# Down-weights in a ring of four and a down-projection two units behind, in a fused gated scan and two MLPs

## Chip, cores and metric

One core of a Trainium2 chip. The metric is the device time of one execution in microseconds (us), as a median of several runs.

## What is computed

```python
# x, f_logit: (1, 6080, 256); lower_bound: (256,)
f = lower_bound + (1 - lower_bound) * sigmoid(f_logit)
for t in range(6080):
    h = f[:, t] * h + (1 - f[:, t]) * x[:, t];  y[:, t] = h
h = y @ w_in1                       # 256 -> 2048
y = maximum(0.01 * h, h) @ w_out1   # leaky, 2048 -> 256
h = y @ w_in2
out = where(h > 0, h, exp(minimum(h, 0)) - 1) @ w_out2   # ELU
```

All of it is float32. The kernel splits each matmul operand in a high and a low part (`_hi`, `_lo`, type fp32r) and makes three matmuls of each product: hi x hi, hi x lo and lo x hi.

## The kernel before

Features lie on the 128 partitions and tokens along the free dimension. The 6080 tokens are cut into 6 pairs of tiles (`PAIRS`); a tile of the first pair has 480 tokens (`N0`), every other one 512 (`BANK`). The 2048 hidden features are 8 pairs of 128-row blocks (`H`, index p). A "step" s multiplies one pair of tiles by one pair of blocks: seven products (Strassen's scheme, `product`) up and eight blocks down (`down11` to `down21`). Steps run over pairs 1 to 5 of the leaky MLP and then over all 6 pairs of the ELU MLP.

The first pair of the first MLP has no steps. Its work is done in 16 **units**, each one tile t and one block pair p, with plain products: `unit_up(i)` is 12 matmuls of 480 columns (2 hidden blocks x 2 feature halves x 3), `unit_down(i)` 12 more into `y_ps`. `unit(i)` gives the order: tile 0 of a block pair comes first and tile 1 two units later, (0,0), (0,1), (1,0), (0,2), (1,1) and so on. TensorE runs `unit_up(i)` and then `unit_down(i-1)`; the last down stands inside step 0, in two halves.

What a unit needs: ACT copies the two PSUM banks to `e` (`unit_pre`), DVE takes the leaky function (`unit_leaky`), ACT writes `g_hi` (`unit_split`), DVE `g_lo` (`g0_ready`). `e`, `g_hi` and `g_lo` have two places, i % 2. ACT's `unit_split(i)` waits for `down0_done >= i - 1`, `unit_up(i)` for the copies of unit i-2.

The weights are split on the way. The raw up-weights of block pair p come to one of three places of `c` (`load_a`), ACT and DVE split them (`split_a`, `a_ready`). The raw down-weights come to the single buffer `w_out_raw` (`load_w_out`), ACT writes `w_out_hi` and DVE `w_out_lo` (`split_w_out`, `w_out_ready`). For the seven products of the steps another load of w_in (`load_w_in`, buffer `w_in_raw`) gets four sums on POOL (`w_sums`) and is split too (`split_w_in`, `w_in_ready`).

All engines are in order. All big loads are issued by SP, in an order written out by hand: `load_w_out(i)` waits for `w_out_ready >= i`, `load_w_in(i)` for `w_in_ready >= i`, `load_a(p)` for `a_ready >= p - 2`; in the loop over i, `load_a(i+1)`, `load_w_out(i)`, `load_w_in(i-2)` follow one another. The scan inputs of pair 1 (`load_scan(1)`) stand ahead of that loop, those of pair 2 (`load_scan(2)`) behind `load_w_in(7)`. On ACT and DVE the small tasks are hung between the unit's own operations in `unit_extra` and `unit_after`, and in a step in `extra`. There, in step 0, ACT has `split_w_in(6)`, `tanh(2,0)`, `tanh(2,1)`, and behind them `split_w(0)` and `copy_sums`, which moves `y_ps` of the first pair to `result`; `down11(0)`, in step 1, waits for that (`y_copied`). The last product of step 0 waits for DVE's `add22`, which stands behind `split11`, and this for the last `unit_down`.

Of the kernel before, what the change touches and what calls it, by code (L numbers as in the profile page):

```python
# [8 lines left out]
def bass_gated_scan__leaky_mlp__elu_mlp(  # L9
# [18 lines left out]
    ALU = mybir.AluOpType  # L28
# [12 lines left out]
    RING = 3  # L41
# [47 lines left out]
    w_in_h, w_out_h = (w_in1, w_in2), (w_out1, w_out2)  # L89

    ctx = ExitStack()
    with ctx:
# [96 lines left out]
        w_out_loaded = sem("w_out_loaded")  # L189
        w_sum_ready = sem("w_sum_ready")  # L190
# [30 lines left out]
        def _(sp):  # L221
# [107 lines left out]
        def _(sc):  # L329
# [22 lines left out]
            def first_gate(n):  # L352
                k, t = FIRST[n]
                f = first_tile(f_in, k, t)
                sc.wait_ge(f0_loaded[n], DMA)
                nc.scalar.activation(f, f, ACT.Tanh, scale=0.5).then_inc(tanh0_ready, 1)
                if n == 0:
                    sc.wait_ge(bound_steps, 2)
                sc.wait_ge(tanh0_ready, n + 1)
                nc.scalar.activation(f, f, ACT.Identity, bias=f_shift[:, k:k + 1], scale=f_scale[:, k:k + 1]  # L360
                                     ).then_inc(forget0_ready, 1)
# [6 lines left out]
            def forget1(k):  # L368
                sc.wait_ge(tanh_ready, k + 1)
# [17 lines left out]
            def split_w_out(i):  # L387
                p = i % H
                sc.wait_ge(w_out_loaded, DMA * (i + 1))
                if i >= H:  # L390
                    sc.wait_ge(out_done, 4 * (LEAKY_STEPS - H + p + 1))
                nc.scalar.copy(w_out_hi[:, p, :], w_out_raw[:, :, :].rearrange("p b c -> p (b c)")
                               ).then_inc(w_out_hi_ready, 1)
# [222 lines left out]
        def _(ve):  # L616
# [503 lines left out]
```

## Time and profile before

| | us |
|---|---|
| median of 3 runs | 1071.63 (1070.43 to 1072.32) |
| the profiled execution | 1072.25 |
| its span | 1070.5 |
| TensorE busy (PE) | 1027.6 (96%) |
| VectorE busy (DVE) | 859.8 (80%) |
| ScalarE busy (ACT) | 620.3 (58%) |

The span runs from the first to the last instruction. PE is TensorE's matmul, PEld its weight load, SP the engine that issues the DMAs. In a row of a timeline the first two numbers are start and duration in us; a bracket at the end tells how long the engine was idle ahead of this operation and who released it. A matmul's duration reaches beyond the start of the next one: the matmuls are pipelined, and the distance of two starts is what one costs.

### The profile page before, as it was taken

What the parts mean: (1) busy time and instruction counts of PE and PEld (TensorE: products, weight loads), DVE (VectorE), ACT (ScalarE), POOL (GpSimd) and SP (SyncE); (2) the same over time, 40 slices, a digit from 0 to 9 for tenths busy, and PEclk for the clock granted to TensorE, in tenths of its full rate; (3) what the DMA queues carried; (4) which work ended last, traced back from release to release, by engine and by line L of the source; (5) the groups of instructions that cost most, each with busy time, mean ns of one, the idle gap of its engine ahead of it and who ended that gap; (6) DMA issues with size and microseconds to landing.
All of it is one profiled execution on the core that took longest, in us unless ns stands there. A gap on an engine that the chain in (4) does not pass through costs nothing.

```text
span 1070.5 us, 12489 instructions
## 1 busy us (share of the span) xinstructions
PE 1027.6 (96%) x4374; PEld 827.3 (77%) x4374; DVE 859.8 (80%) x1118; ACT 620.3 (58%) x953; POOL 43.2 (4%) x69
## 2 busy tenths in 40 slices
PE   8778869999999999999999999999999999999997
PEld 5667648878878887887887888888888888888886
DVE  6356658878888888887999888888888888888775
ACT  5443544554464554455667766767676666666564
POOL 0011200000000000000431000000000000000000
PEclk9899879999999999999999999999999999999999
DMA  4321030030030021010213011011011001001001
GB/s 128 123 59 50 20 126 1 1 118 0 1 118 1 1 79 40 1 57 18 82 59 99 1 40 38 1 40 40 1 40 40 1 27 52 1 1 40 1 1 39
DMA packets 24814, 42.41 MB, mean 40 GB/s; under 512 B 2224, under 2 KB 13488, under 8 KB 24752
## 3 DMA queue, kind: packets, MB, share of 16 engines
q1 hardware_dynamic: 24176, 41.36, 11.4%
q8 instruction: 34, 0.56, 0.2%
q10 hardware_dynamic: 576, 0.26, 0.1%
q14 instruction: 28, 0.23, 0.1%
HBM read 29.16 MB, written 12.45 MB: 39 GB/s over the span
## 4 chain that ended last, share of the span: by engine, by line
PE 84%; DVE 2%; DMA 1%; ACT 1%; issue 0%; SPq 0%; DVEq 0%; ACTq 0%
PE y_ps L967 15%; PE y_ps L969 15%; PE y_ps L968 15%; PE a_ps L958 7%; PE a_ps L960 7%; PE a_ps L959 7%; PE c_ps L960 4%; PE c_ps L958 4%; PE c_ps L959 4%; PE b_ps L960 2%; PE b_ps L958 2%; PE b_ps L959 2%; DMA f_in<-f_logitT 1%; ACT g_hi L487 0%; DVE g_lo L793 0%
## 5 line engine op out<-in xcount | busy, mean ns | idle before, releaser
L967 PE MATMUL y_ps<-g_hi,w_out_hi 128*128 128x512 f32 (+1 forms) x768 | 307.9, 401 | 33.0 <-DVE g_lo L650 19.0
L968 PE MATMUL y_ps<-g_lo,w_out_hi 128*128 128x512 f32 (+1 forms) x768 | 305.7, 398 | 0.0
L969 PE MATMUL y_ps<-g_hi,w_out_lo 128*128 128x512 f32 (+1 forms) x768 | 305.3, 397 | 0.0
L967 PEld LDWEIGHTS y_ps<-g_hi,w_out_hi 128*128 128x128 f32 x768 | 146.8, 191 | 72.9 <-DVE g_lo L650 24.0
L969 PEld LDWEIGHTS y_ps<-g_hi,w_out_lo 128*128 128x128 f32 x768 | 147.0, 191 | 33.7
L968 PEld LDWEIGHTS y_ps<-g_lo,w_out_hi 128*128 128x128 f32 x768 | 147.0, 191 | 32.4
L487 ACT CAST g_hi<-e 128x1024 fp32r<-128x1024 f32 (+1 forms) x88 | 92.1, 1046 | 113.4 <-DVE e L774 111.3
L958 PE MATMUL a_ps<-x_hi,w_in_hi 128*128 128x512 f32 (+1 forms) x352 | 139.3, 396 | 2.7 <-DVE c L736 2.7
L960 PE MATMUL a_ps<-x_hi,w_in_lo 128*128 128x512 f32 (+1 forms) x352 | 139.1, 395 | 0.0
L959 PE MATMUL a_ps<-x_lo,w_in_hi 128*128 128x512 f32 (+1 forms) x352 | 139.1, 395 | 0.0
L793 DVE TENSOR_TENSOR g_lo<-e,g_hi 128x1024 fp32r<-128x1024 f32 (+1 forms) x88 | 107.8, 1225 | 7.0 <-ACT g_hi L487 2.2
L454 ACT ACTIVATE e<-c 128x1024 f32<-128x1024 f32 (+1 forms) x48 | 50.6, 1053 | 75.9 <-DVE c L731 70.1
L438 ACT COPY c<-c_ps 128x512 f32<-128x512 f32 (+1 forms) x88 | 51.4, 584 | 61.5 <-PE c_ps L960 61.5
L726 DVE TENSOR_TENSOR c<-c,b_ps 128x512 f32<-128x512 f32 (+1 forms) x88 | 60.2, 684 | 33.2 <-PE b_ps L960 32.6
L789 DVE TENSOR_TENSOR g_lo<-e,g_hi 128x512 fp32r<-128x512 f32 (+1 forms) x88 | 61.3, 696 | 30.0 <-ACT g_hi L479 30.0
L731 DVE TENSOR_TENSOR c<-c,c_ps 128x512 f32<-128x512 f32 (+1 forms) x88 | 60.3, 685 | 29.1 <-PE c_ps L960 28.9
L958 PEld LDWEIGHTS a_ps<-x_hi,w_in_hi 128*128 128x128 f32 x352 | 66.5, 189 | 18.5 <-DVE c L736 3.1
L960 PEld LDWEIGHTS a_ps<-x_hi,w_in_lo 128*128 128x128 f32 x352 | 66.5, 189 | 15.6
L959 PEld LDWEIGHTS a_ps<-x_lo,w_in_hi 128*128 128x128 f32 x352 | 66.5, 189 | 15.4
L960 PE MATMUL c_ps<-x_hi,w_in_lo 128*128 128x512 f32 (+1 forms) x176 | 69.6, 395 | 0.0
L958 PE MATMUL c_ps<-x_hi,w_in_hi 128*128 128x512 f32 (+1 forms) x176 | 69.6, 395 | 0.0
L959 PE MATMUL c_ps<-x_lo,w_in_hi 128*128 128x512 f32 (+1 forms) x176 | 69.5, 395 | 0.0
(94 smaller groups left out, 1502.0 us busy)
## 6 DMA issues: line engine op xcount, KB each, us to landing
f_in<-f_logitT SPq DMA_DIRECT2D x10, 512.0 KB, 4.9
x_in<-xT SPq DMA_DIRECT2D x10, 512.0 KB, 6.1
mid<-result SPq DMA_DIRECT2D x10, 512.0 KB, 3.5
x_in<-mid SPq DMA_DIRECT2D x5, 1024.0 KB, 5.0
outT<-result SPq DMA_DIRECT2D x10, 512.0 KB, 2.8
w_out_raw<-w_out SPq DMA_DIRECT2D x16, 256.0 KB, 3.1
w_in_raw<-w_in SPq DMA_DIRECT2D x32, 128.0 KB, 2.3
f_in<-f_logitT SPq DMA_DIRECT2D x4, 240.0 KB, 5.0
```

The lines of the kernel that those rows point to most:

```text
L438: nc.scalar.copy(c[:, 2, cols(s)], c_ps[:, cols(s)]).then_inc(snap5_ready, 1)
L487: nc.scalar.copy(g_hi[:, 1:3, cols(s)], e[:, 1:3, cols(s)]).then_inc(hi_w_ready, 1)
L726: nc.vector.tensor_tensor(c[:, 0, cols(s)], c[:, 0, cols(s)], b_ps[:, cols(s)], ALU.add).then_inc(c11_ready, 1)
L731: nc.vector.tensor_tensor(c[:, 1, cols(s)], c[:, 1, cols(s)], c_ps[:, cols(s)], ALU.add).then_inc(c12_ready, 1)
L789: nc.vector.tensor_tensor(g_lo[:, 0, cols(s)], e[:, 0, cols(s)], f32_view(g_hi[:, 0, cols(s)]), ALU.subtract).then_inc(g11_ready, 1)
L793: nc.vector.tensor_tensor(g_lo[:, 1:3, cols(s)], e[:, 1:3, cols(s)], f32_view(g_hi[:, 1:3, cols(s)]), ALU.subtract).then_inc(g_w_ready, 1)
L958: nc.tensor.matmul(out, w_in_hi[:, p, at], hi, start=start, stop=False, skip_group_check=not start)
L959: nc.tensor.matmul(out, w_in_hi[:, p, at], lo, start=False, stop=False, skip_group_check=not start)
L960: return nc.tensor.matmul(out, w_in_lo[:, p, at], hi, start=False, stop=True, skip_group_check=not start)
L967: nc.tensor.matmul(out, w_out_hi[:, p, at], hi, start=(p == 0 and j == 0), stop=False)
L968: nc.tensor.matmul(out, w_out_hi[:, p, at], lo, start=False, stop=False)
L969: last = nc.tensor.matmul(out, w_out_lo[:, p, at], hi, start=False, stop=(p == H - 1 and j == 1))
```

## The change

The raw down-weights of the first MLP get four places in `result` (`OUT_RING`, `raw_out`), which holds nothing until the first sums are copied; these copies now also wait for `w_out_ready >= 8`. SP issues loads 0 to 3 at once and 4 to 7 as places come free, and `load_a` ahead of `load_scan(1)` as far as block pair 6; `load_w_in(7)` goes behind `load_scan(2)`. The order of the units puts tile 0 two units further ahead. `unit_down` comes two units behind `unit_up`, so that the last two stand in step 0. The gate of the first pair (`Identity` with scale and bias) moves from ACT to DVE (`first_forget`), and the small tasks of the first units are ordered anew.

```diff
-    RING = 3
+    RING, OUT_RING = 3, 4
 def unit(i):
-        if i == 0:
-            return 0, 0
-        if i == UNITS - 1:
-            return 1, H - 1
-        return (0, (i + 1) // 2) if i % 2 else (1, i // 2 - 1)
+        if i < 3:
+            return 0, i
+        if i >= UNITS - 3:
+            return 1, i - H
+        return (1, (i - 3) // 2) if i % 2 else (0, i // 2 + 1)
+        def raw_out(i):
+            return result[:, i % OUT_RING // 2, i % 2, :] if i < H else w_out_raw[:, :, :].rearrange("p b c -> p (b c)")
 # SP: load_w_out
-                if i > 0:
+                raw = raw_out(i).rearrange("p (b c) -> p b c", c=D)
+                if i < H:
+                    if i >= OUT_RING:
+                        sp.wait_ge(w_out_ready, i - OUT_RING + 1)
+                    sp.dma_start(raw, w_out1[:, 2 * p:2 * p + 2, :]).then_inc(w_out0_loaded[i % OUT_RING], DMA)
+                else:
                     sp.wait_ge(w_out_ready, i)
-                sp.dma_start(w_out_raw[:, :, :], w_out_h[m][:, 2 * p:2 * p + 2, :]).then_inc(w_out_loaded, DMA)
+                    sp.dma_start(raw, w_out2[:, 2 * p:2 * p + 2, :]).then_inc(w_out_loaded, DMA)
 # SP: order of the loads, behind load_w_out(1)
+            load_w_out(2)
+            load_w_out(3)
+
+            load_a(3)
+            load_a(4)
+            load_w_out(4)
+            load_a(5)
+            load_w_out(5)
+            load_a(6)
             load_scan(1)
+            load_w_out(6)
             load_w_in(0)
-            for i in range(2, H):
-                if i + 1 < H:
-                    load_a(i + 1)
-                load_w_out(i)
-                if i > 2:
-                    load_w_in(i - 2)
-            load_w_in(H - 2)
-            load_w_in(H - 1)
+            load_a(7)
+            load_w_out(7)
+            for i in range(1, H - 1):
+                load_w_in(i)
 # ... and behind load_scan(2), ahead of store(0)
+                if r == 1:
+                    load_w_in(H - 1)
 # ACT: the start
-            first_gate(0)
-            first_gate(1)
+            first_tanh(0)
+            first_tanh(1)
+            first_split(0)
             split_a(0)
-            first_split(0)
-            first_gate(2)
+            first_tanh(2)
+            split_a(1)
             first_split(1)
-            split_a(1)
-            first_gate(3)
+            first_tanh(3)
 # DVE: the gate
+                nc.vector.tensor_scalar(f, f, f_scale[:, k:k + 1], f_shift[:, k:k + 1],
+                                        ALU.mult, ALU.add).then_inc(forget0_ready, 1)
 # ACT: unit_extra (split_a and split_w_out on DVE likewise)
                 if i == 0:
+                    split_a(2)
                     split_w_out(0)
+                if i == 1:
                     first_split(2)
-                elif i == 1:
                     first_split(3)
                     split_w_out(1)
-                    split_a(2)
-                elif i % 2 and (i + 3) // 2 < H:
-                    split_a((i + 3) // 2)
-                elif i % 2 == 0 and i // 2 + 1 < H:
+                    split_a(3)
+                if i == 2:
+                    split_w_out(2)
+                if i >= 3 and i % 2 and (i + 5) // 2 < H:
+                    split_a((i + 5) // 2)
+                if i >= 4 and i % 2 == 0 and i // 2 + 1 < H:
                     split_w_out(i // 2 + 1)
 # DVE: unit_after
                 if i == 0:
                     split_w_out(0)
+                    first_forget(3)
+                    first_input(3)
                     scan(0, 1, 1)
                     first_split(2)
+                    first_split(3)
                 if i == 1:
-                    first_split(3)
+                    split_a(3)
                     save_carry(0)
-                    split_w_out(1)
-                    split_a(2)
+                if i == 2:
+                    split_w_out(2)
 # ACT and DVE, extra(s) and copy_sums(0)
-                if s < 2:
-                    split_w_in(H - 2 + s)
+                if s in (0, 2):
+                    split_w_in(H - 2 + s // 2)
                 if r == 0:
                     sc.wait_ge(down0_done, units_through(t, H - 1))
+                    sc.wait_ge(w_out_ready, H)
 # TensorE: step 0, between A12 and S1; and the loop over the units
                 else:
+                    unit_down(UNITS - 2, (0, 1))
                     pe.wait_ge(pre0, 2 * UNITS)
-                if i > 0:
-                    unit_down(i - 1, (0, 1))
+                if i > 1:
+                    unit_down(i - 2, (0, 1))
```

## Rows read from the trace of the kernel before

**Rows 1.** Stretches: us, then busy us (and count) of each engine, granted clock, DMA

```profile
11.43:125.44 114.01, 92.42 (x372) 76.14 (x373) 66.14 (x73) 52.26 (x82) 12.15 (x24) 0.90 0.20 61
39.42:42.62 3.20, 3.20 (x9) 2.64 (x8) 2.21 (x3) 1.47 (x2) 0.00 (x0) 0.50 0.04 16
125.44:159.19 33.75, 22.05 (x80) 17.01 (x79) 17.42 (x23) 12.78 (x20) 3.98 (x8) 0.80 0.31 107
159.19:1070.40 911.21, 904.38 (x3895) 730.76 (x3893) 771.13 (x1015) 548.36 (x843) 26.33 (x32) 1.00 0.09 32
```

**Rows 2.** Timeline of TensorE without waits; 98.06 to 105.03 is 32 starts

```profile
98.06 0.38 PE L989 MATMUL a_ps<-x_hi,w_in_lo 128*128 128x480 f32 x1
...
105.03 0.38 PE L988 MATMUL c_ps<-x_lo,w_in_hi 128*128 128x480 f32 x1
...
158.49 0.40 PE L958 MATMUL a_ps<-x_hi,w_in_hi 128*128 128x512 f32 x1
...
159.19 0.39 PE L958 MATMUL a_ps<-x_hi,w_in_hi 128*128 128x512 f32 x1
```

**Rows 3.** Timeline of TensorE, units: four of its six restarts after a wait

```profile
19.22 0.67 PE L967 MATMUL y_ps<-g_hi,w_out_hi 128*128 128x480 f32 x1 [2.12 <-DVE w_out_lo L655]
...
38.85 0.77 PE L967 MATMUL y_ps<-g_hi,w_out_hi 128*128 128x480 f32 x1 [6.74 <-DVE g_lo L650]
...
80.64 0.71 PE L967 MATMUL y_ps<-g_hi,w_out_hi 128*128 128x480 f32 x1 [2.09 <-DVE g_lo L650]
...
94.91 0.49 PE L967 MATMUL y_ps<-g_hi,w_out_hi 128*128 128x480 f32 x1 [1.91 <-DVE g_lo L650]
```

**Rows 4.** Timeline of TensorE, steps 0 and 1: its restarts after a wait

```profile
135.11 0.61 PE L958 MATMUL a_ps<-x_hi,w_in_hi 128*128 128x512 f32 x1 [2.69 <-DVE c L736]
...
148.04 0.77 PE L967 MATMUL y_ps<-g_hi,w_out_hi 128*128 128x512 f32 x1 [9.01 <-ACT result L504]
```

**Rows 5.** Waits, 0 to 110 us: engine and operation, releaser, us, times, longest

```profile
ACT w_out_hi L392 <- DMA w_out_raw<-w_out: 27.5, 5, 8.6
```

**Rows 6.** Waits of SP's queue, 0 to 120 us

```profile
SPq L258 <- DVE w_in_lo L621: 70.0, 5, 20.4
```

**Rows 7.** Groups by line, 0 to 160 us: count, busy, mean ns, idle

```profile
L967 PE MATMUL y_ps<-g_hi,w_out_hi 128*128 128x480 f32 x64 | 28.9, 451 | 21.2 <-DVE g_lo L650 19.0 <-DVE w_out_lo L655 2.1
...
L650 DVE TENSOR_TENSOR g_lo<-e,g_hi 128x960 fp32r<-128x960 f32 x16 | 18.9, 1178 | 11.7 <-ACT g_hi L385 11.7
L646 DVE SCALAR_TENSOR_TENSOR e<-e 128x960 f32<-128x960 f32 x16 | 18.5, 1154 | 12.4 <-ACT e L379 12.4
...
L385 ACT CAST g_hi<-e 128x960 fp32r<-128x960 f32 x16 | 15.9, 992 | 10.9 <-DVE e L646 10.9
...
L379 ACT COPY e<-a_ps 128x480 f32<-128x480 f32 x16 | 8.9, 555 | 15.8 <-PE a_ps L989 15.8
...
L655 DVE TENSOR_TENSOR w_out_lo<-w_out_raw,w_out_hi 128x512 fp32r<-128x512 f32 x8 | 5.5, 690 | 24.1 <-ACT w_out_hi L392 24.1
...
L360 ACT ACTIVATE f_in<-f_in,f_shift,f_scale 128x480 f32<-128x480 f32 x4 | 3.2, 788 | 0.2
...
L691 DVE TENSOR_TENSOR_SCAN x_in<-f_in,carry,x_in 128x512 f32<-128x512 f32 x2 | 2.6, 1278 | 0.0
...
L661 DVE TENSOR_SCALAR f_in<-f_in,f_scale,f_shift 128x1024 f32<-128x1024 f32 x2 | 1.6, 810 | 6.1 <-ACT f_in L398 6.1
```

**Rows 8.** Loads of f issued at 25.62, 137.91, 138.84: KB, us to landing

```profile
f_in<-f_logitT SPq DMA_DIRECT2D x1, 512.0 KB, 7.1
...
f_in<-f_logitT SPq DMA_DIRECT2D x1, 512.0 KB, 4.1
...
f_in<-f_logitT SPq DMA_DIRECT2D x1, 512.0 KB, 5.7
```

**Rows 9.** Timeline of ACT in step 0

```profile
142.01 1.06 ACT L398 ACTIVATE f_in<-f_in 128x1024 f32<-128x1024 f32 x1 [7.19 <-DMA f_in<-f_logitT]
...
146.47 1.47 ACT L504 COPY result<-y_ps 128x480 f32<-128x480 f32 x3
```

More of the change, by code:

```diff
@@ L88, in bass_gated_scan__leaky_mlp__elu_mlp @@
     mid_h = mid.rearrange("(k p) s -> p k s", p=P)
-    w_in_h, w_out_h = (w_in1, w_in2), (w_out1, w_out2)
+    w_in_h = (w_in1, w_in2)
     ctx = ExitStack()
@@ L189, in bass_gated_scan__leaky_mlp__elu_mlp @@
         w_out_loaded = sem("w_out_loaded")
+        w_out0_loaded = [sem(f"w_out0_loaded{n}") for n in range(OUT_RING)]
         w_sum_ready = sem("w_sum_ready")
@@ L350, in split_a, with first_tanh @@
                 nc.scalar.copy(w_in_hi[:, p, 0:4 * P], c[:, p % RING, :]).then_inc(a_hi_ready, 1)
-            def first_gate(n):
-                k, t = FIRST[n]
-                f = first_tile(f_in, k, t)
+            def first_tanh(n):
+                f = first_tile(f_in, *FIRST[n])
                 sc.wait_ge(f0_loaded[n], DMA)
                 nc.scalar.activation(f, f, ACT.Tanh, scale=0.5).then_inc(tanh0_ready, 1)
[L357 to L361, printed above, removed]
             def first_split(n):
@@ L368, in forget1 @@
             def forget1(k):
+                if k == 0:
+                    sc.wait_ge(bound_steps, 2)
                 sc.wait_ge(tanh_ready, k + 1)
@@ L388, in split_w_out @@
                 p = i % H
-                sc.wait_ge(w_out_loaded, DMA * (i + 1))
-                if i >= H:
+                if i < H:
+                    sc.wait_ge(w_out0_loaded[i % OUT_RING], DMA * (i // OUT_RING + 1))
+                else:
+                    sc.wait_ge(w_out_loaded, DMA * (i - H + 1))
                     sc.wait_ge(out_done, 4 * (LEAKY_STEPS - H + p + 1))
-                nc.scalar.copy(w_out_hi[:, p, :], w_out_raw[:, :, :].rearrange("p b c -> p (b c)")
-                               ).then_inc(w_out_hi_ready, 1)
+                nc.scalar.copy(w_out_hi[:, p, :], raw_out(i)).then_inc(w_out_hi_ready, 1)
             def tanh(r, k):
@@ L598, in _ @@
                 unit_pre(i, 1)
-                if i != 1:
-                    unit_extra(i)
+                unit_extra(i)
                 unit_split(i)
-                if i == 1:
-                    unit_extra(i)
             for s in range(STEPS):
@@ L627, in split_a, with first_forget @@
                                         ALU.subtract).then_inc(a_ready, 1)
+            def first_forget(n):
+                k, t = FIRST[n]
+                f = first_tile(f_in, k, t)
+                ve.wait_ge(tanh0_ready, n + 1)
+                nc.vector.tensor_scalar(f, f, f_scale[:, k:k + 1], f_shift[:, k:k + 1],
+                                        ALU.mult, ALU.add).then_inc(forget0_ready, 1)
             def first_input(n):
@@ L654, in split_w_out @@
                 ve.wait_ge(w_out_hi_ready, i + 1)
-                nc.vector.tensor_tensor(w_out_lo[:, i % H, :], w_out_raw[:, :, :].rearrange("p b c -> p (b c)"),
+                nc.vector.tensor_tensor(w_out_lo[:, i % H, :], raw_out(i),
                                         f32_view(w_out_hi[:, i % H, :]), ALU.subtract).then_inc(w_out_ready, 1)
@@ L801, in copy_sums @@
                     ve.wait_ge(down0_done, units_through(0, H - 1))
+                    ve.wait_ge(w_out_ready, H)
                 else:
@@ L808, in extra @@
                 r, p = pair_of(s)
-                if s < 2:
-                    split_w_in(H - 2 + s)
+                if s in (0, 2):
+                    split_w_in(H - 2 + s // 2)
                 if r == PAIRS - 1 and p >= 2:
@@ L883, in unit_extra @@
                 if i == 0:
-                    first_input(3)
-                elif i % 2 and i >= 3 and (i + 3) // 2 < H:
-                    split_a((i + 3) // 2)
-                elif i % 2 == 0 and i // 2 + 1 < H:
+                    split_a(2)
+                if i == 1:
+                    split_w_out(1)
+                if i >= 3 and i % 2 and (i + 5) // 2 < H:
+                    split_a((i + 5) // 2)
+                if i >= 4 and i % 2 == 0 and i // 2 + 1 < H:
                     split_w_out(i // 2 + 1)
@@ L922, in _ @@
             ve.wait_ge(bound_steps, 2)
+            first_forget(0)
             first_input(0)
             scan(0, 0, 0)
+            first_forget(1)
             first_input(1)
+            first_split(0)
             scan(0, 1, 0)
             split_a(0)
-            first_split(0)
             first_split(1)
             split_a(1)
+            first_forget(2)
             first_input(2)
```

## Prediction

> **What bounds the kernel now.** I read three views in turn. First the stretches [rows 1]: from 159.19 us on, TensorE is busy 904.4 of 911.2 us at full clock, and its work there is the same after the change, so there is nothing to win in it. Ahead of it, the loop over the 16 units of the first pair (11.43 to 125.44) runs at a mean clock of 0.90 and steps 0 and 1 (to 159.19) at 0.80. Everything must come out of these 148 us.
>
> Second, the work in them. A 480-column matmul takes 6.97/32 = 0.218 us where nothing waits, a 512-column one 0.70/3 = 0.233 us [rows 2]. There are 16 units x 24 = 384 of the first kind and 21 + 21 + 24 = 66 of the second ahead of the start of step 2: 84.0 + 15.4 = 99.4 us. The kernel takes 159.19 - 11.43 = 147.8 us, so 48.4 us are lost. In the unit loop the first down matmuls wait 21.2 us in all [rows 7], in six waits, four of them 2.12, 6.74, 2.09 and 1.91 us [rows 3]; in steps 0 and 1 TensorE waits 2.69 and 9.01 us [rows 4]: 32.9 us. The rest, some 15 us, is half clock (the 3.20 us after one of these waits, at clock 0.50 [rows 1]) and small spaces.
>
> Third, who is late. The releaser named is mostly DVE's g_lo, but the chain behind it starts at the raw down-weights: ACT waits 27.5 us, five times, for w_out_raw [rows 5], and ACT is in order, so the next g_hi stands behind it. The load is late because it stands in SP behind load_w_in, which waits 70 us in all for w_in_ready [rows 6]; so w_out comes a round of two units late. In step 1 the 9.01 us end with ACT's copy of the sums [rows 4], which stands behind tanh(2,0) and tanh(2,1); ACT waits 7.19 us there for f of pair 2 [rows 9], a load that stands in SP behind load_w_in(7), and that waits for DVE's S-weight split in step 0.
>
> **The change, part by part.** I walk the new order with durations of [rows 7] and 0.22/0.23 us a matmul; a half unit (12 matmuls) is 2.63 us. Where an engine's operations follow one another, the next begins 0.1 us before the end shown.
>
> *Start.* Four gates leave ACT (0.79 us each [rows 7]) and come to DVE. No row shows this DVE operation at 480 columns. The nearest row is the same operation at 1024, 0.81 us: by columns alone that is 0.38 us, the lower end; the upper is ACT's own 0.79 us. I take 0.47 us, close to the row of the same operation. DVE does two gates ahead of TensorE's first operand, and the first has room, so the ends move the start by -0.1 to +0.3 us. Gate, input and scan then end at 6.9 us (k=0) and 10.3 (k=1), the split of x k=0 at 9.2, w_in_lo(0) at 10.9, x k=1 at 11.9 us. TensorE starts at 11.0 instead of 11.43: gain 0.4 us.
>
> *Units 0 to 2.* up(0) ends at 14.0, up(1) at 16.6 us. up(2) is now tile 0, pair 2, and needs w_in_lo(2): ACT copies at 14.7 (after the two pre copies), DVE at 15.9, ready 16.55: no wait. The raw weights are issued ahead of the three new w_out loads (768 KB). Three loads of 512 KB took 0.9 + 7.1 = 8 us from the first issue [rows 8], 5 us a MB, so if all three shared the way with them and held them up, it would be by up to 3.9 us, of which about 2 are spare; I take nothing, and 2 us as the upper end. g(0) is ready at 18.2 us, w_out_lo(0) at 18.8; down(0) runs from 19.3, behind up(2): the 2.12 us wait has cover.
>
> *Unit 3 (tile 1, pair 0).* DVE: gate(3), input(3), scan end at 21.1, ACT's two x copies 21.7, x_lo 22.4 us: up(3), from 22.0 to 24.6, finds them. But ACT waited for the scan in front of w_out(1) and g(1), and DVE for ACT: leaky(1) ends at 23.5, g_hi 24.5, g_lo 25.7 us. down(1) starts at 25.7 instead of 24.6: **a wait of 1.1 us is left**.
>
> *Units 4 and 5, and pair 1's loads.* SP now issues load_scan(1) behind load_a(6), which waits for w_in_lo(3) (26.3 us): at 27.8 instead of 24.8. Its f lands 4.1 to 7.1 us after issue; 4.1 is a first f behind a weight load [rows 8], 7.1 a second f, and I take 4.1 for the first: 31.9. ACT, in order, does tanh(1,0) ahead of g(3): free at 33.0, g_lo(3) at 35.2 us. down(3) is due behind up(5) at 36.3: covered by 1.1 us. The same for g(4), which has tanh(1,1) ahead of it: 39.6 against 41.6 us.
>
> *Units 6 to 15.* The loads of w_out have left the loop: 0 to 3 are there at the start, 4 to 7 are issued as soon as a ring place is free, at least one round ahead. load_w_in no longer has a w_out behind it; w_in_ready to landing and the four POOL sums take 5 us of the 10.5 us of a round. What is new is that ACT's g copy of unit i waits for down(i-2), which on TensorE is now behind up(i); queued behind that wait are the pre copies of unit i+1. From the end of down(i-2): g_hi 0.99 + g_lo 1.18 = 2.2 us; TensorE has up(i+1), down(i-1), up(i+2) = 7.9 us first. DVE has in a round of two units 2 leaky, 2 g_lo, a split of w_in_lo, w_out_lo and S-weights, and at most 2 scans: 2 x 1.15 + 2 x 1.18 + 3 x 0.69 + 2 x 1.28 = 9.3 of 10.5 us. So from 25.7 us TensorE goes through: up(15) ends at 88.8, down(13) at 91.5.
>
> *Steps 0 and 1.* Step 0 gets 12 matmuls more (down(14)), the loop has 12 fewer. Its last product waits as before for split11(0), which stands behind the last down: the 2.69 us of [rows 4] stay, from 101.0 to 103.7, with 9 matmuls at half clock (1.7 us) as now. The sums: S-weights of pair 5 are ready at 95.6; SP issues w_in(6) and then pair 2's f at once, with no w_in(7) between. f lands at 96.5 + 4.1 = 100.6 and 97.4 + 5.7 = 103.1 us [rows 8]; tanh ends 104.2, split_w(0) (waits for DVE's leaky, 105.0) 106.0, the three copies (1.47 us [rows 9]) 107.4. TensorE arrives there at 107.5: the 9.01 us go, and the half clock behind them. The new wait for all 8 w_out in the sums costs nothing: the last is at 76 us. Step 2 starts at 116.7 us.
>
> **Sum.** Left are 0.3 us at the start, 1.1, 2.7, 1.7 and some 0.5 us: 6.3 instead of 48.4. With the earlier start: 42.1 + 0.4 = 42.5 us = 159.2 - 116.7. The span would be 1028.0 us. The profiled run took 1072.25 us with a span of 1070.5, 0.6 over the median of 1071.63: the median becomes **1029.1 us**.
>
> *The clock.* After the waits of 2.12 and 2.09 us the first matmul took 0.67 and 0.71 us (half clock), after that of 1.91 us 0.49 us [rows 3]; so I give the 1.1 us none, and the 2.7 us one. The Trainium skill, "TensorE: Matmul & The Clock Gate", in its Part 1 on the clock gate, says that the monitor runs free of the kernel, so that the place of the change varies from run to run. By this either wait could be followed by half clock or not: by the 1.7 us that the row gives, the sum would be 1027.4 or 1030.8 us.
>
> **Rivals.**
> 1. *A wait takes the place* (chance 0.24). The first f of pair 1 lands at 7.1 us, not 4.1: ACT's tanh(1,0) moves g_lo(3) to 38.2, TensorE waits 1.9 us, and half clock adds 1.7: 1032.7. If the second f of pair 2 or a w_out is late too, the step-1 wait is back in part: 9.0 us whole would make 1038 to 1042. For it: ACT stands in order behind every load, three engines pass work in a ring, and my slack is 1.1 us at two places. Against: the landings of [rows 8].
> 2. *It doesn't do what it says* (0.05): the ring moves the lateness of w_out to the loads behind it in SP (load_a, load_w_in, load_scan(1)), so only half of the loop's gain and none of step 1's comes: 1071.6 - 17 = 1055. Against: w_out_ready(1) and (2), for which SP waits, are there at 19 and 24 us.
> 3. *Slower* (0.02): the two g buffers close the ring. If g(i), waiting for down(i-2), set the start of the next unit, all is in a row: 5.26 + pre 0.56 + 1.15 + 0.99 + 1.18 = 9.1 us a unit. 14 units make 128 us, with 5 for the rest 133 against 80.5 forecast: 1082 us. It is slower from 8.3 us a unit. Against: the 7.9 us of cover above.
> 4. The forecast (0.67): 1026 to 1032. Another hang-up, one that I don't see, has 0.02.
>
> **How the numbers follow.** Low end: the wait of 1.1 us and the half clock of 1.7 us both stay away (waits of 1.91 us went without it): 1029.1 - 2.8 = 1026.3, and 0.3 for the spread of the runs: 1026. High end: rival 1 reaches 1038 with all but a few hundredths of its chance; above it lie a small part of rival 1, rivals 2 and 3 and the unseen, some 0.13. About 0.2% (2 us) is what a measurement of this kernel tells from no change. Faster 0.96 (the forecast and rivals 1 and 2), same 0.01 and slower 0.03 (rival 3's 0.02 and the unseen 0.02, shared).
>
> **What would show it.** Right: ACT's w_out_hi no longer waits for DMA; start of step 2 near 117; one TensorE wait of about 1 us near 25 and one of 2.7 near 101; clock 1.00 in the loop. Wrong: a TensorE restart between 28 and 90 us (rival 1: behind tanh f_in near 35; rival 3: in every unit with ACT's g_hi released by TensorE just before), or a restart with releaser ACT result in step 1.

## The result, and the profile after

| | before | changed |
|---|---|---|
| median, us | 1071.03 (1067.97 to 1072.32) | 1038.37 (1036.98 to 1040.19) |
| profiled execution, us | 1072.25 | 1039.38 |
| its span, us | 1070.5 | 1037.6 |

The ratio is 0.970, with a 95% interval of 0.9672 to 0.9728: 32.7 us gained where 42.5 were forecast, and 0.4 us above the upper end of the range, 1038.0. The profiled execution lies 1.0 us above the median. The stretches of the changed kernel, in the columns of [rows 1] (stretch in us, its length, then busy us and count of TensorE, weight loads, VectorE, ScalarE and POOL, granted clock, share and GB/s of DMA):

```profile
10.83:25.47 14.64, 13.58 (x60) 10.90 (x61) 13.43 (x18) 8.95 (x16) 0.00 (x0) 1.00 0.40 131
25.47:98.90 73.43, 71.50 (x321) 59.80 (x321) 55.80 (x58) 40.28 (x64) 22.91 (x24) 1.00 0.21 67
98.90:125.70 26.80, 18.98 (x68) 14.71 (x69) 17.27 (x22) 12.19 (x19) 3.92 (x8) 0.87 0.39 135
125.70:1037.60 911.90, 904.80 (x3896) 730.66 (x3894) 770.95 (x1016) 548.79 (x845) 28.02 (x32) 1.00 0.09 32
```

The long last stretch is as it was [rows 1]. The clock of the unit loop has gone from 0.90 to 1.00, and the waits for w_out_raw of [rows 5] are gone. What is missing lies ahead of 125.96 us, the start of step 2, which was forecast for 116.7. TensorE's timeline shows where it waits; these answer to [rows 3, 4]:

```profile
25.47 0.48 PE L1000 MATMUL y_ps<-g_hi,w_out_hi 128*128 128x480 f32 x1 [1.06 <-DVE g_lo L673]
...
89.58 0.49 PE L1000 MATMUL y_ps<-g_hi,w_out_hi 128*128 128x480 f32 x1 [0.49 <-DVE g_lo L673]
...
95.21 0.48 PE L1000 MATMUL y_ps<-g_hi,w_out_hi 128*128 128x480 f32 x1 [1.32 <-DVE g_lo L673]
...
100.30 0.50 PE L991 MATMUL a_ps<-x_hi,w_in_hi 128*128 128x512 f32 x1 [1.52 <-ACT c L448]
...
108.19 0.50 PE L991 MATMUL a_ps<-x_hi,w_in_hi 128*128 128x512 f32 x1 [2.88 <-DVE c L759]
...
114.09 0.77 PE L1000 MATMUL y_ps<-g_hi,w_out_hi 128*128 128x512 f32 x1 [3.54 <-ACT result L520]
```

The first and the fifth were forecast (1.1 and 2.7 us). The other four were not, 6.87 us together. Behind the last the clock is at its lower level: 0.77 us for the first matmul, and 14 starts from 114.09 to 120.16 take 6.07 us where 14 x 0.233 = 3.26 would do, 2.8 us more.

Who is late is seen in SP's timeline. It issues each load of the weights for the seven products (the S-weights, `w_in_raw`) once the last ones are split. Here is the first issue of three of these loads, and behind the last the issue of f for pair 2:

```profile
44.55 0.33 SPq L263 DMA_DIRECT2D w_in_raw<-w_in  x1
...
56.29 0.33 SPq L263 DMA_DIRECT2D w_in_raw<-w_in  x1
...
102.72 0.33 SPq L263 DMA_DIRECT2D w_in_raw<-w_in  x1
...
103.62 0.41 SPq L235 DMA_DIRECT2D f_in<-f_logitT  x1
```

The first three rounds, to 79.60, are 11.7 us each, the next one 12.3 and the one behind it 10.8; TensorE's round of two units is 10.5. Pair 2's f is issued at 103.6, forecast for 96.5. One round in full, from the load at 44.55 to the next at 56.29, in three timelines. POOL, the four sums:

```profile
47.28 0.85 POOL L335 TENSOR_TENSOR w_in_raw<-w_in_raw 128x128 f32<-128x128 f32 x1 [7.94 <-DMA w_in_raw<-w_in]
48.09 1.44 POOL L336 TENSOR_TENSOR w_in_raw<-w_in_raw 128x128 f32<-128x128 f32 x1
49.49 1.37 POOL L338 TENSOR_TENSOR w_in_raw<-w_in_raw 128x128 f32<-128x128 f32 x1
50.95 0.79 POOL L340 TENSOR_TENSOR w_in_raw<-w_in_raw 128x128 f32<-128x128 f32 x1
```

ACT, the cast of the sums and the g_hi behind it:

```profile
51.77 0.62 ACT L359 CAST w_in_hi<-w_in_raw 128x512 fp32r<-128x512 f32 x1 [3.71 <-POOL w_in_raw L340]
52.30 0.99 ACT L399 CAST g_hi<-e 128x960 fp32r<-128x960 f32 x1
```

And VectorE:

```profile
47.73 1.49 DVE L694 SCALAR_TENSOR_TENSOR x_in<-f_in,x_in 128x1024 f32<-128x1024 f32 x1
49.14 1.41 DVE L669 SCALAR_TENSOR_TENSOR e<-e 128x960 f32<-128x960 f32 x1
50.47 0.94 DVE L642 TENSOR_TENSOR w_in_lo<-c,w_in_hi 128x512 fp32r<-128x512 f32 x1
53.32 1.16 DVE L673 TENSOR_TENSOR g_lo<-e,g_hi 128x960 fp32r<-128x960 f32 x1 [1.90 <-ACT g_hi L399]
54.40 1.28 DVE L714 TENSOR_TENSOR_SCAN x_in<-f_in,carry,x_in 128x512 f32<-128x512 f32 x1
55.59 0.67 DVE L637 TENSOR_TENSOR w_in_lo<-w_in_raw,w_in_hi 128x512 fp32r<-128x512 f32 x1
```

Add it up. Issue to first sum is 2.7 us and the sums are 4.5 us (47.28 to 51.74). From there through cast, g_hi, g_lo and scan to the end of the split it is 4.5 us more: 11.7. The ring closes because the split on VectorE, for which SP waits, stands behind the g_lo and the scan, and g_hi on ACT behind the cast that waits for the sums. That is also how TensorE comes to feel it: ACT stands still for 3.71 us in front of the cast, and g_hi with it. The durations of POOL's rows are rough by nature, but the distances of their starts say the same.

The sums are not always slow. The set that meets an idle VectorE (its timeline is empty from 111.3 to 114.5) takes 0.45 us for each, 1.8 us in all; the first two:

```profile
112.84 0.45 POOL L335 TENSOR_TENSOR w_in_raw<-w_in_raw 128x128 f32<-128x128 f32 x1 [5.06 <-DMA w_in_raw<-w_in]
113.25 0.46 POOL L336 TENSOR_TENSOR w_in_raw<-w_in_raw 128x128 f32<-128x128 f32 x1
```

### The profile page after: what moved, and what is told of

The parts are those of the page before. It is cut to its first block, busy times and chain, and to the rows that moved or that the text cites. A ratio compares the mean times of both kernels' runs of the same rounds, so it can differ in the third digit from the quotient of the medians.

```text
span 1037.6 us, 12494 instructions
## 1 busy us (share of the span) xinstructions
PE 1016.8 (98%) x4374; PEld 819.3 (79%) x4374; DVE 863.5 (83%) x1122; ACT 615.4 (59%) x949; POOL 55.6 (5%) x69
## 3 DMA queue, kind: packets, MB, share of 16 engines
q1 hardware_dynamic: 24176, 41.36, 11.6%
## 4 chain that ended last, share of the span: by engine, by line
PE 86%; DVE 4%; DMA 3%; ACT 2%; POOL 2%; issue 2%; SPq 1%; ACTq 0%; DVEq 0%
PE y_ps L1000 16%; PE y_ps L1002 15%; PE y_ps L1001 15%; PE a_ps L993 8%; PE a_ps L991 8%; PE a_ps L992 8%; PE c_ps L993 4%; PE c_ps L991 4%; PE c_ps L992 4%; PE b_ps L993 2%; PE b_ps L991 2%; PE b_ps L992 2%; DMA f_in<-f_logitT 1%; DMA w_in_raw<-w_in 1%; ACT g_hi L399 1%
## 5 line engine op out<-in xcount | busy, mean ns | idle before, releaser
L1000 PE MATMUL y_ps<-g_hi,w_out_hi 128*128 128x512 f32 (+1 forms) x768 | 303.7, 395 | 9.3 <-ACT result L520 3.5
L1001 PE MATMUL y_ps<-g_lo,w_out_hi 128*128 128x512 f32 (+1 forms) x768 | 302.1, 393 | 0.0
L1002 PE MATMUL y_ps<-g_hi,w_out_lo 128*128 128x512 f32 (+1 forms) x768 | 301.9, 393 | 0.0
L1000 PEld LDWEIGHTS y_ps<-g_hi,w_out_hi 128*128 128x128 f32 x768 | 144.6, 188 | 47.4 <-DVE g_lo L816 5.4
L1002 PEld LDWEIGHTS y_ps<-g_hi,w_out_lo 128*128 128x128 f32 x768 | 144.7, 188 | 33.2
L1001 PEld LDWEIGHTS y_ps<-g_lo,w_out_hi 128*128 128x128 f32 x768 | 144.7, 188 | 32.4
L502 ACT CAST g_hi<-e 128x1024 fp32r<-128x1024 f32 (+1 forms) x88 | 92.0, 1046 | 111.3 <-DVE e L797 109.2
L993 PEld LDWEIGHTS a_ps<-x_hi,w_in_lo 128*128 128x128 f32 x352 | 66.3, 188 | 15.5
```

Of the source, the lines that this page charges most:

```text
L502: nc.scalar.copy(g_hi[:, 1:3, cols(s)], e[:, 1:3, cols(s)]).then_inc(hi_w_ready, 1)
L993: return nc.tensor.matmul(out, w_in_lo[:, p, at], hi, start=False, stop=True, skip_group_check=not start)
L1000: nc.tensor.matmul(out, w_out_hi[:, p, at], hi, start=(p == 0 and j == 0), stop=False)
L1001: nc.tensor.matmul(out, w_out_hi[:, p, at], lo, start=False, stop=False)
L1002: last = nc.tensor.matmul(out, w_out_lo[:, p, at], hi, start=False, stop=(p == H - 1 and j == 1))
```

## The experiments

The kernel before has a median of 1070.11, 1070.34 or 1070.76 us in the series that the ratios below are taken from. All diffs are against the changed kernel, but for the one said; "..." marks lines left out. The expectations name their own theories. The main question is why the round took 11.7 us, and whether this ring and nothing else held back the 9.3 us by which the median (1038.37) missed the forecast (1029.1).

**The length of the sums.**

```diff
+                n_cols = P if i >= H else 1
-                a21, a11, a12, a22 = (w_in_raw[:, n, :] for n in range(4))
+                a21, a11, a12, a22 = (w_in_raw[:, n, 0:n_cols] for n in range(4))
...
```

The other columns of the sums hold a constant: their values are left out.

> The changed kernel with POOL's four sums of the first eight w_in loads over one column instead of 128 (the rest of the sum blocks is a constant, so this part of the products is left out in value, not in work). Theory A: in the loop over the units the S-weights form a ring of load (2.7 us), four sums (4.5), ACT's and DVE's splits with g_hi, g_lo and a scan between them (4.5), 11.7 us against TensorE's 10.5 for two units, and the sums are 4.5 instead of 1.9 us because POOL and DVE block each other. Then the ring falls to about 8 us, DVE's stretched operations get their normal length, the TensorE waits at 89, 95 and 99 us vanish, pair 2's f comes some 6 us earlier: step 2 starts near 117, about 1030 us. Theory B: the three engines together, not the sums, are at their limit there, or the load is: 1036 to 1039.

Measured: 1032.71 us (1030.94 to 1034.42), ratio 0.9649 (0.9636 to 0.9663). POOL's timeline, one set:

```profile
48.27 0.57 POOL L337 TENSOR_TENSOR w_in_raw<-w_in_raw 128x1 f32<-128x1 f32 x1 [9.97 <-DMA w_in_raw<-w_in]
48.80 1.18 POOL L338 TENSOR_TENSOR w_in_raw<-w_in_raw 128x1 f32<-128x1 f32 x1
49.93 1.11 POOL L340 TENSOR_TENSOR w_in_raw<-w_in_raw 128x1 f32<-128x1 f32 x1
51.12 0.52 POOL L342 TENSOR_TENSOR w_in_raw<-w_in_raw 128x1 f32<-128x1 f32 x1
```

A sum over one column still takes up to 1.18 us here, and 0.19 us in the set at 37.55, which meets an idle VectorE: most of a slow sum is waiting, not adding. VectorE's timeline shows for what:

```profile
48.71 1.22 DVE L698 SCALAR_TENSOR_TENSOR x_in<-f_in,x_in 128x1024 f32<-128x1024 f32 x1
49.84 1.15 DVE L673 SCALAR_TENSOR_TENSOR e<-e 128x960 f32<-128x960 f32 x1
50.91 0.69 DVE L646 TENSOR_TENSOR w_in_lo<-c,w_in_hi 128x512 fp32r<-128x512 f32 x1
```

The last three sums end at 49.98, 51.04 and 51.64 us, these operations at 49.93, 50.99 and 51.60: each sum ends with the VectorE operation beside it. VectorE's operations have their normal length, as expected.

The set takes 3.4 us instead of 4.5, and the first three rounds 10.5 to 10.7 (not the 8 expected: 2.7 + 3.4 + 4.5 = 10.6). 5.7 us of the 9.3 come back. The wait of 1.06 us at 25 is the only one left in the unit loop. Pair 2's f is issued at 99.3, still 2.8 us later than forecast, and the step-1 wait is still 3.32 us.

**The load ahead of the split.** `load_w_in(i)` waits for the sums instead of the split, and POOL for the split of the last set, so the load lies beside the chain on ACT and VectorE.

```diff
-                if i > 0:
+                if 0 < i < H:
+                    sp.wait_ge(w_sum_ready, 4 * i)
+                elif i >= H:
                     sp.wait_ge(w_in_ready, i)
 # POOL, w_sums(i)
+                if 0 < i < H:
+                    po.wait_ge(w_in_ready, i)
```

> The changed kernel, but load_w_in(i) for i under 8 waits only for the sums of i-1 (which have read the raw blocks), and POOL waits for the split of i-1 before it writes the sums of i: all work is done, the load leaves the ring. Theory A: ring 11.7 - 2.7 = 9.0 us, under 10.5, though each set of sums stays at about 4.5 us: 1029 to 1031 us. Theory C (it is DVE itself that is stretched by POOL, 0.2 to 0.3 us for each operation that meets a sum, and that sets the pace): no gain, 1037 to 1039 us, while the short sums gain.

Measured: 1029.53 us (1026.83 to 1030.84), ratio 0.9618 (0.9602 to 0.9633): within 0.5 us of the time forecast for the change. The sums are as slow as ever, 4.9 us for this set of four; POOL's timeline now shows VectorE as the releaser of the first:

```profile
44.63 1.24 POOL L339 TENSOR_TENSOR w_in_raw<-w_in_raw 128x128 f32<-128x128 f32 x1 [5.54 <-DVE w_in_lo L641]
...
48.18 1.32 POOL L344 TENSOR_TENSOR w_in_raw<-w_in_raw 128x128 f32<-128x128 f32 x1
```

But they are no longer in a row with 2.7 us of load: SP issues at 39.12, 49.53, 59.51, 69.49, 79.28 and 89.61, pair 2's f at 94.59, and TensorE has two waits left, the two that were forecast:

```profile
25.15 0.48 PE L1004 MATMUL y_ps<-g_hi,w_out_hi 128*128 128x480 f32 x1 [1.05 <-DVE g_lo L677]
...
101.43 0.61 PE L995 MATMUL a_ps<-x_hi,w_in_hi 128*128 128x512 f32 x1 [2.68 <-DVE c L763]
```

So opening the ring brings back 8.8 of the 9.3 us, the whole of the miss within the spread of the runs. (The trace is of the fastest execution, 1026.83 us; its step 2 starts at 114.54, where 116.7 was forecast.) VectorE's own lengthened operations can't be the cause by themselves, for they are still there (1.49 us for the input product at 47.70).

**The split ahead of the scan.** The other link of the same ring: VectorE's `split_w_in` moves from behind the scan (1.28 us) to ahead of it.

```diff
+                if i >= 5 and i % 2:
+                    split_w_in((i - 5) // 2)
                 if i in (5, 6):
                     scan_input(1, i - 5)
...
-                if i >= 5 and i % 2:
-                    split_w_in((i - 5) // 2)
```

> The changed kernel, but DVE's S-weight split stands ahead of the scan work in unit_after, not behind it. Theory A: the ring is 1.3 to 1.5 us shorter, 10.3 us, just under TensorE's 10.5: most of the lateness goes, 1031 to 1033 us. Theories B and C: nothing changes, 1037 to 1039.

Measured: 1030.89 us (1030.41 to 1032.87), ratio 0.9637 (0.9624 to 0.965). The first rounds are 10.1 to 10.9 us (44.11, 54.38, 64.49, 75.37), the next 12.0. In the loop only a wait of 0.34 us is left beside that at 25, in step 0 one of 2.68, in step 1 one of 1.40. Its time can't be told from that of the last experiment: either link, taken out, opens the ring for the most part. The link on ACT, the cast ahead of g_hi, was not moved in any run.

**One POOL operation for four.**

```diff
+                if i < H:
+                    nc.gpsimd.tensor_tensor(w_in_raw[:, 4:8, :], w_in_raw[:, 0:4, :], w_in_raw[:, 0:4, :], ALU.add).then_inc(w_sum_ready, 1)
+                    return
...
```

As many elements are read and written, but these are not the four sums: their values are left out.

> The changed kernel with POOL's four sums of 128 columns replaced, for the first eight loads, by one operation over all 512 (as many elements in and out, but not the four sums: their values are left out). The short sums of the run before still took 3.3 us a set, so it is each operation's wait for DVE that costs, not its length. Theory A: one operation waits once, 1.8 us of its own and up to 1.2 of waiting: 3 us a set, ring 10.2 us, under 10.5: 1030 to 1032 us. Rival (POOL's rate is halved while DVE works, whatever the number of operations): 4.5 us a set and 1037 to 1039 us.

Measured: 1032.77 us (1029.93 to 1034.36), ratio 0.9648 (0.9628 to 0.9668). One set in POOL's timeline, and the VectorE operation beside it:

```profile
47.13 1.44 POOL L336 TENSOR_TENSOR w_in_raw<-w_in_raw 128x512 f32<-128x512 f32 x1 [9.74 <-DMA w_in_raw<-w_in]
...
47.59 2.06 DVE L698 SCALAR_TENSOR_TENSOR x_in<-f_in,x_in 128x1024 f32<-128x1024 f32 x1
```

The same 512 columns in one instruction take 1.44 us and not 4.5 (1.04 us in the set at 36.35, which meets an idle VectorE), half of the 3 us expected: the price hangs on the number of instructions. VectorE pays for the long instruction: its input product takes 2.06 us instead of 1.22. The first two rounds are 10.3 us (44.41, 54.75, 65.07), as TensorE's two units make them, the next 10.8 and 11.5. The time is still 3.2 us above that of the early load. TensorE waits 3.41 us at the end of step 0 and 1.04 us in step 1, and behind these waits 17 matmuls in all run at half clock.

**The sums on VectorE.** What the slow sums wait for.

```diff
...
+                if i >= 5 and i % 2:
+                    w_sums((i - 5) // 2)        # now on VectorE
                 unit_leaky(i)
 # POOL
-            for i in range(2 * H):
+            for i in range(H - 2, 2 * H):
```

> The four sums of the S-weights of units 0 to 5 of that load (block pairs 0 to 5) go from POOL to VectorE, ahead of its leaky function of every second unit; nothing else is changed. Theory A (POOL and VectorE hold each other up, operation by operation): with POOL idle in the loop VectorE's operations are back at their own length, the input product 1.22 us instead of 1.49, the leaky function 1.15 instead of 1.41, w_in_lo 0.68 instead of 0.94; a set of sums takes VectorE some 1.0 to 1.2 us (a 128x512 operation takes 0.69 and a 128x960 one 1.16, so 128 columns some 0.2 to 0.3 each), the load of the next S-weights comes every 10.5 us as TensorE sets it, VectorE is close to full (9.3 + 1.1 of 10.5 us), and the time is 1028 to 1033 us. Rival (the long operations come from something else, the loads or the order of work): the same three VectorE operations still take 1.4 to 1.5 and 0.94 us with POOL idle, and the 1.1 us more make the loop wait as now or more, 1038 to 1042 us.

Measured: 1033.16 us (1030.89 to 1035.82), ratio 0.9649 (0.9627 to 0.967), just above the 1033 of theory A. VectorE's timeline at the place shown above:

```profile
47.59 1.22 DVE L705 SCALAR_TENSOR_TENSOR x_in<-f_in,x_in 128x1024 f32<-128x1024 f32 x1
48.72 0.28 DVE L637 TENSOR_TENSOR w_in_raw<-w_in_raw 128x128 f32<-128x128 f32 x1
48.93 0.29 DVE L638 TENSOR_TENSOR w_in_raw<-w_in_raw 128x128 f32<-128x128 f32 x1
49.13 0.28 DVE L640 TENSOR_TENSOR w_in_raw<-w_in_raw 128x128 f32<-128x128 f32 x1
49.45 0.29 DVE L642 TENSOR_TENSOR w_in_raw<-w_in_raw 128x128 f32<-128x128 f32 x1
49.66 1.15 DVE L680 SCALAR_TENSOR_TENSOR e<-e 128x960 f32<-128x960 f32 x1
50.73 0.69 DVE L653 TENSOR_TENSOR w_in_lo<-c,w_in_hi 128x512 fp32r<-128x512 f32 x1
```

With POOL idle the three operations of VectorE are back from 1.49, 1.41 and 0.94 to 1.22, 1.15 and 0.69 us, and a whole set of sums takes 1.0 us. This is the other half of the proof: the stretched operations of VectorE and the slow sums on POOL go together. VectorE takes the additional work without a wait of TensorE between 25.06 and 103.6 us, so it isn't the bound of the loop either. At 103.6 it waits 2.83 us, with half clock behind. Between its median and that of the kernel with the early load (1029.53) lie 3.6 us; later rounds here are 10.9 and 11.6 us long (65.30, 76.20, 87.80), in which VectorE also has the sums and the split of x for pair 1.

**The ring of four alone.** The kernel before, with its own order of units, with `OUT_RING` = 4 and the loads of w_out two earlier; ACT keeps the gate, and down stays one unit behind.

```diff
+            load_w_out(2)
+            load_w_out(3)
             for i in range(2, H):
                 if i + 1 < H:
                     load_a(i + 1)
-                load_w_out(i)
+                if i + 2 < H:
+                    load_w_out(i + 2)
...
```

> The kernel before with the ring of four alone (loads two pairs ahead of their use in the old order; old order of units, down-projection one unit behind, gate on ACT). ACT's 27.5 us of waits for w_out should go. If the lateness of w_out is the main loss in the loop, it takes most of the loop's 21 us of waits and their half clock: about 1045. The S-weight ring of theory A holds here too and one unit of cover is short of the chain pre, leaky, g_hi, g_lo with small tasks between them, so I expect less, about 1052; and the 9 us wait in step 1 stays.

Measured: 1051.03 us (1050.79 to 1052.12), ratio 0.9824 (0.981 to 0.9837), as expected. By itself the ring is worth 19.1 of the 32.7 us. ACT's waits for the load of w_out are gone. TensorE's timeline keeps seven waits of 0.4 to 2.1 us in the loop, and the wait of [rows 4] in step 1 is untouched:

```profile
127.54 0.76 PE L983 MATMUL y_ps<-g_hi,w_out_hi 128*128 128x512 f32 x1 [9.14 <-ACT result L519]
```

Its S-weights, too, come every 11.7 us (50.44, 62.17, 73.85), with sums of up to 1.45 us: as soon as w_out is out of the way, the ring of the S-weights is what the loop waits for.

**Down one unit behind.** All of the change but that.

```diff
-                    unit_down(UNITS - 2, (0, 1))
...
-                if i > 1:
-                    unit_down(i - 2, (0, 1))
+                if i > 0:
+                    unit_down(i - 1, (0, 1))
```

> The changed kernel with the down-projection one unit behind again, all else as changed. From the end of an up half to its g_lo it takes pre 0.6, leaky 1.2, g_hi 1.0, g_lo 1.2 and the small tasks between them, 4.5 to 7 us, against 5.26 us until TensorE wants it. If the two units are what the change lives on, TensorE waits 1 us or more in nearly every unit: 1048 to 1055. If the ring of four and the order of tile 0 carry it: 1039 to 1043.

Measured: 1041.79 us (1040.82 to 1042.48), ratio 0.9733 (0.9718 to 0.9749). The cover of down two units behind is worth 3.4 us, the difference of the medians, as long as the ring of the S-weights is closed: its rounds are 11.7 us here too (48.05, 59.80, 71.47, 83.17), and no run prices the cover with the ring open. Since the ring of four alone gives 1051.03 us, the 9.2 us between the two kernels belong to the order of the units and loads and to the gate on VectorE; no run takes these apart. TensorE waits 2.14 us at 18.42, the wait of 2.12 us of [rows 3] that two units of distance cover in the change, and then 0.6 to 1.1 us in each round.

**The copies of the sums in step 0**, ahead of the S-weights and of tanh(2,k), so that they no longer stand behind pair 2's load.

```diff
+                if s == 0:
+                    copy_sums(0, 1, 0)
+                    copy_sums(0, 1, 1)
...
-                if s % H == 0:
+                if s % H == 0 and s > 0:
...
```

> The changed kernel, but in step 0 ACT copies the first pair's sums right behind split11 and S-weight split 6, ahead of tanh(2,0) and tanh(2,1), and DVE its quarter ahead of leaky. The wait of 3.54 us in step 1 and the 15 matmuls at half clock behind it (2.9 us) go, the waits at 89 to 100 us stay. This prices the tail alone: 1032 to 1033 us. If something else than the copies holds step 1, 1037 to 1039.

Measured: 1036.19 us (1033.8 to 1037.31), ratio 0.9678 (0.966 to 0.9697). This is a miss: 2.2 us came of the 5 to 6 expected. The wait for the result is gone, and one of 0.68 us (g_lo) stands in its place. The waits of the loop and of the first product of step 0 are there as before (1.07, 1.36 and 1.47 us). But part of the half clock has only moved: behind the wait of 2.79 us in step 0, where the change kept full clock, nine starts from 109.05 to 112.69 take 3.6 us where 2.1 would do. Another part of the difference is the spread: this trace is of an execution of 1033.8 us, 2.4 below the median.

**Split 11 one place earlier.**

```diff
-                    sc.wait_ge(down0_done, UNITS)
+                    sc.wait_ge(down0_done, UNITS - 1)
```

> One number: ACT's cast of g_hi of product 11 of step 0 waits for 15 instead of all 16 down-projections of the first pair (its place in the buffer is free by then), so that TensorE's wait of 2.88 us at the end of step 0 has nothing to wait for. Theory A (pair 2's load sets the copies in step 1, whatever TensorE does ahead of it): the 2.88 us go, TensorE comes to the sums some 2.5 us sooner and waits there that much longer, about 6 us with ACT result as releaser; the time stays at 1037 to 1039 us. Rival (each wait counts for itself): the wait in step 1 stays at 3.5 us and the time falls by 2.5 to 3 us to some 1035.5 us.

Measured: 1038.12 us (1037.1 to 1039.86), ratio 0.9692 (0.9679 to 0.9705), so no change. The wait at the end of step 0 falls from 2.88 to 1.34 us, and that in step 1 grows from 3.54 to 5.13:

```profile
116.33 0.77 PE L1000 MATMUL y_ps<-g_hi,w_out_hi 128*128 128x512 f32 x1 [5.13 <-ACT result L520]
```

What sets the copies is not what the expectation named, though. ACT's timeline shows that in this run it is the S-weights that stand ahead of tanh:

```profile
111.40 0.62 ACT L359 CAST w_in_hi<-w_in_raw 128x512 fp32r<-128x512 f32 x1 [4.54 <-POOL w_in_raw L340]
```

Pair 2's f had landed by then, as both tanh follow without a wait. Both loads are issued late by SP, the S-weights at 104.91 us and f at 105.81.

**All three together**: the load ahead of the split, the copies in step 0 and split 11 earlier.

> All work done: load_w_in after the sums, copies early, and ACT's split11 of step 0 waits for the 15th down unit only, whose g it overwrites, instead of all 16. Against the load after the sums (1029.5) the wait of 2.7 us at the end of step 0 and its half clock of up to 1.7 us go: 1025 to 1027 us. If the step-0 wait only moves to the next product or to step 1: 1028 to 1030.

Measured: 1027.36 us (1026.39 to 1027.74), ratio 0.9598 (0.9582 to 0.9613), the lowest median here and 0.4 us above what was expected. The stretches:

```profile
10.80:98.90 88.10, 87.03 (x397) 73.72 (x396) 74.69 (x82) 53.75 (x85) 26.67 (x28) 1.00 0.29 92
98.90:113.58 14.68, 12.94 (x56) 9.91 (x54) 12.12 (x17) 8.10 (x12) 2.14 (x4) 1.00 0.44 166
```

The clock is 1.00 throughout, and three waits are left, 1.07 us at 25.21, 0.72 at 105.21 and 1.02 at 107.19. The wait of 2.68 us at the end of step 0, which the kernel with the early load had, is gone. It is the one that the earlier split 11 is meant for, so this edit, worth nothing by itself, seems to pay once nothing else stands behind it in step 1. That isn't shown: no run has it with the early load alone, and the 2.2 us between the two medians are about the spread of the runs.

## Why the prediction was partly right

The change was read rightly up to 45 us, and the gain has the sign and the places forecast. Step by step:

1. *Start.* VectorE's gate at 480 columns took 0.53 us (0.47 taken, bounds 0.38 to 0.79), and TensorE began at 10.83 us (11.0).
2. *Units 0 to 2.* No wait of TensorE; the three additional loads held up nothing that it needed. *Unit 3*: a wait of 1.06 us at 25.47 (1.1 at 25.7).
3. *Units 4 and 5.* load_scan(1) was issued at 27.44 (27.8), its f landed 3.8 us later, at 31.27 (31.9), and g_lo(3) ended at 34.4 (35.2). This was the trigger of rival 1, and it didn't come.
4. *Units 6 to 15.* **This is the step that failed.** It said that "w_in_ready to landing and the four POOL sums take 5 us of the 10.5 us of a round". They took 2.7 + 4.5 = 7.2 us: the 5 us are what load and sums take while VectorE is idle (58.24 to 62.76 in the kernel before, 4.5 us). And the sum stopped there: that the split waits behind cast, g_hi, g_lo and scan, another 4.5 us, so that the ring has 11.7 and not 5 us, was left out. Either slip alone was enough to hide the bound: the whole ring with fast sums is 2.7 + 1.8 + 4.5 = 9.0 us, and load and sums alone, with slow sums, are 7.2, both under 10.5. Only the whole ring with slow sums, 11.7, shows it. "So from 25.7 us TensorE goes through" rests on this step. The kernel with the early load takes the ring apart with the slow sums in it and comes to 1029.53 us.
5. *Steps 0 and 1.* The wait of 2.7 us came (2.88), and the clock stayed at 1.00 up to the next wait. The copies ended at 114.0 and not at 107.4, because pair 2's f was issued 7.1 us late, at the end of the slow rounds; that gave the 3.54 us and the half clock behind them.

| loss ahead of step 2, us | forecast | measured |
|---|---|---|
| wait at 25 us | 1.1 | 1.06 |
| waits of the loop behind it | 0 | 0.49 + 1.32 |
| first wait of step 0 | 0 | 1.52 |
| end of step 0 | 2.7 | 2.88 |
| step 1 | 0 | 3.54 |
| half clock | 1.7 | 2.8 |
| small spaces and the start | 0.8 | 2.1 |
| sum | 6.3 | 15.7 |

The last line is 125.96 - 10.83 - 99.4 = 15.7. With the start 0.2 us earlier, the difference of 9.4 is that of 9.3 us between the medians forecast and measured. The 99.4 us of work have a slip: 384 x 6.97/32 us is 83.6 and not 84.0, so that 0.4 us more belong to the small spaces, in both columns. And the third rival is slower from 8.4 us a unit on, (80.5 + 42.5 - 5)/14, and not from 8.3. Neither moves the forecast.

Two of the prediction's own signs of being wrong appeared: a restart of TensorE between 28 and 90 us (0.49 us at 89.58), and one with the releaser ACT result in step 1.

Of the rivals, the first had the size (a wait in step 1, 1038 to 1042 us) and the place, and named "three engines pass work in a ring" in its favour. But neither of the causes that it gave came: the loads took about as long as forecast once issued (pair 2's second f 6.1 us against 5.7). So its upper figure is met by another mechanism. The second and third didn't come: ACT has no wait for w_out, and its waits for g_hi in the loop (15.5 us, eight of them) all end with VectorE's e and none with `down0_done`.

The warning stood in the trace of before. Its sets at 34.8, 60.9, 75.2 and 89.6 us fall where VectorE is idle, and each sum takes 0.45 to 0.46 us; the sixth, at 120 us, meets VectorE's g_lo, which takes 1.47 us there instead of the mean 1.18 of [rows 7]. POOL's timeline of the kernel before:

```profile
121.03 1.38 POOL L320 TENSOR_TENSOR w_in_raw<-w_in_raw 128x128 f32<-128x128 f32 x1
122.49 0.79 POOL L322 TENSOR_TENSOR w_in_raw<-w_in_raw 128x128 f32<-128x128 f32 x1
```

Of the clock: a wait of 2.68 us at the same place in TensorE's program was followed by a first matmul of 0.61 us in the kernel with the early load (clock 0.56 in the 2 us behind it) and by one of 0.50 in that with short sums, where the lower level came later (0.80 in the 2 us behind it). The change itself kept 1.00 behind its 2.88 us, so the 1.7 us forecast for this place didn't come, and 2.8 us did in step 1. The Trainium skill says in "TensorE: Matmul & The Clock Gate", Part 1, that the monitor runs free of the kernel, and the two waits of 2.68 us agree with it.

## What to carry to other kernels

A buffer that is loaded, worked on by several engines and then loaded again is a ring: add up all of it, from the issue to the semaphore that allows the next issue, with everything that stands in order ahead of each link, and compare the whole with the round of the bounding engine. Take the durations from a moment that is as crowded as the one to be predicted: removing one bottleneck makes the other engines meet. If the ring is too long, look first at what it waits for and in which order. Waiting only for the last reader that really holds the buffer (here the load needs only the sums to be done), or moving one operation out from ahead of a link, gave 1029.5 and 1030.9 us with all work done. Speeding up the sums, with their values left out, gave 1032.7 and 1032.8.

## What the runs showed of the hardware

POOL and VectorE hold each other up, operation by operation:

| on POOL, two SBUF operands | VectorE idle | beside VectorE | VectorE's operation beside it |
|---|---|---|---|
| 128x1 | 0.19 us | up to 1.18 | not longer (1.22) |
| 128x128 | 0.45 | mostly 0.8 to 1.5 | 0.2 to 0.3 longer (1.49) |
| 128x512 | 1.04 | 1.44 | 0.8 longer (2.06) |

In brackets is VectorE's input product of 1024 columns, which takes 1.22 us with POOL idle. The clearest row is one of the second MLP in the changed kernel, where VectorE goes from one operation to the next from 475.29 to 477.7 us and then has a gap of 0.45 us:

```profile
475.24 2.79 POOL L335 TENSOR_TENSOR w_in_raw<-w_in_raw 128x128 f32<-128x128 f32 x1 [26.18 <-DMA w_in_raw<-w_in]
477.99 0.46 POOL L336 TENSOR_TENSOR w_in_raw<-w_in_raw 128x128 f32<-128x128 f32 x1
```

The sum ends in that gap. The Trainium skill, "SBUF — State Buffer", section "SBUF: two separate sides", says that the two engines share a pair of ports as "an exclusive lock, not a bandwidth split", also against VectorE operations with two SBUF inputs, and that the one that comes second waits for the whole instruction. The rows agree with it: the single-column sums end with the VectorE operations beside them, the delay of VectorE grows with the length of POOL's instruction, and the long sum above ends in the gap. Beside an operation of VectorE with one operand in PSUM the sums weren't held up (0.18 us at 102.60 in the run with short sums, beside `c<-c,c_ps`). What no run here separates is how long POOL can be passed over: in the row above it was for three operations of VectorE, in the unit loop mostly for one.

Waits of TensorE and the clock behind them, from the timelines of all kernels run: the first matmul was at the lower level (0.76 to 0.79 us) after waits of 3.32, 3.33, 3.41, 3.54, 4.48, 5.13, 6.74, 9.01 and 9.14 us. It was not after the 3.79 us that end at 66.19 in the kernel before: the first took 0.48 us, and the lower level came 0.8 us later. After waits of 2.1 to 2.9 us all of this was seen: a first matmul of 0.67 and 0.71 us after 2.12 and 2.09 us [rows 3], one of 0.45 after 2.14 us with clock 1.00 behind it, in others the lower level within 1.6 us, and clock 1.00 up to the next wait after 2.88 us.
